# The last matmul of a feed-forward chain, with its operands' roles exchanged: 9 matmuls of 512 columns become 12 of 384

## What is computed

```python
def _moe2_ref(x, w1, w2, w3, w_out):      # x 3072 x 384, w1 and w2 384 x 1024
    a = x @ w1
    b = x @ w2
    h = a * b @ w3                        # w3 1024 x 1024
    return (h @ w_out).astype(np.float32) # w_out 1024 x 384
```

## Time and profile before

| | |
|---|---|
| median of 3 runs | 1001.33 us (1001.08 to 1002.03) |
| the profiled execution | 1001.33 us |
| its span, first to last instruction | 999.6 us |
| TensorE matmuls, busy | 903.1 us, 90% of the span, 5298 matmuls |
| VectorE, ScalarE, GpSimd busy | 608.0, 427.8, 70.0 us |
| the last block, from its first matmul to the end of the span | 700.9 to 999.6 us |

### The profile page before, as it was taken

One profiled execution on the slowest core, in us unless ns is written; L12 is line 12 of the kernel. 1 busy time (PEld: TensorE's weight loads), 2 busy tenths in 40 slices (PEclk: granted clock), 3 DMA queues, 4 the chain that ended last, 5 costly groups with the idle time before them and its releaser, 6 DMA issues.

```text
span 999.6 us, 14220 instructions
## 1 busy us (share of the span) xinstructions
PE 903.1 (90%) x5298; PEld 807.0 (81%) x5298; DVE 608.0 (61%) x974; ACT 427.8 (43%) x612; POOL 70.0 (7%) x56
## 2 busy tenths in 40 slices
PE   0964839999999899999899999988999999999998
PEld 0533739889989899899899999988788888888887
DVE  5977878989898898899899733345221212121211
ACT  3152264574674664764764654667011111112111
POOL 0000000000000000000000000000222222222221
PEclk9995669999999999999999999999999999999999
DMA  9666066273381470570660540142101010101000
GB/s 337 233 199 180 20 193 128 96 173 89 117 199 45 140 204 13 155 192 14 176 170 12 152 103 11 33 167 78 34 1 64 1 63 0 63 0 64 1 32 32
DMA packets 97878, 99.50 MB, mean 100 GB/s; under 512 B 6928, under 2 KB 88848, under 8 KB 97808
## 3 DMA queue, kind: packets, MB, share of 16 engines
q1 hardware_dynamic: 97808, 98.59, 34.5%
HBM read 63.96 MB, written 29.88 MB: 94 GB/s over the span
## 4 chain that ended last, share of the span: by engine, by line
PE 62%; DVE 22%; DVEq 6%; ACT 4%; issue 3%; DMA 2%; ACTq 1%; SPq 0%
PE ps_p L1285 8%; PE ps_p L1286 7%; PE ps_p L1287 7%; PE ps L1285 7%; PE ps L1287 7%; PE ps L1286 7%; PE ps_ay L1321 3%; DVE sp L1166 3%; DVE an L998 2%; PE ps_ay L1285 2%; PE ps_ay L1287 2%; PE ps_ay L1286 2%; PE ps_k L1285 2%; PE ps_k L1287 2%; PE ps_k L1286 2%
## 5 line engine op out<-in xcount | busy, mean ns | idle before, releaser
L1285 PE MATMUL ps_p<-x1h,win_h 128*128 128x384 f32 x336 | 118.3, 352 | 20.1 <-DVE sp L1166 20.1
L629 POOL TENSOR_TENSOR abl<-ab,abh 128x512 fp32r<-128x512 f32 x48 | 69.0, 1438 | 922.7 <-DVE abh L1267 922.7
L1285 PE MATMUL ps<-g_h,wo_h 128*128 128x384 f32 x384 | 132.3, 345 | 0.0
L1287 PE MATMUL ps<-g_h,wo_l 128*128 128x384 f32 x384 | 129.0, 336 | 0.0
L1286 PE MATMUL ps<-g_l,wo_h 128*128 128x384 f32 x384 | 128.8, 335 | 0.0
L1286 PE MATMUL ps_p<-x1l,win_h 128*128 128x384 f32 x336 | 114.0, 339 | 0.0
L1287 PE MATMUL ps_p<-x1h,win_l 128*128 128x384 f32 x336 | 113.9, 339 | 0.0
L1321 PE MATMUL ps_ay<-stq,stk 96*128 96x128 f32 x384 | 56.7, 295 | 37.5 <-DVE am L1120 15.2
L745 ACT ACTIVATE g_h<-sp 128x768 fp32r<-128x768 f32 (+1 forms) x71 | 55.4, 781 | 74.1 <-DVE sp L1166 74.1
L1258 DVE TENSOR_TENSOR ab<-ps_ay,bc 128x512 f32<-128x512 f32 x24 | 16.6, 692 | 114.6 <-ACT bc L894 114.6
L1321 PEld LDWEIGHTS ps_ay<-stq,stk 96*128 96x128 f32 x384 | 54.0, 208 | 38.8 <-issue 23.1
(11 more groups left out here) (140 smaller groups left out, 1997.2 us busy)
## 6 DMA issues: line engine op xcount, KB each, us to landing
qk_scr<-tt SPq DMA_DIRECT2D x16, 576.0 KB, 4.6
stq<-qk_scr SPq DMA_DIRECT2D x48, 192.0 KB, 4.9
qk_scr<-pp SPq DMA_DIRECT2D x16, 576.0 KB, 4.2
stk<-qk_scr SPq DMA_DIRECT2D x48, 192.0 KB, 4.6
an<-in_a_re SPq DMA_DIRECT2D x8, 576.0 KB, 4.1
an<-in_a_im SPq DMA_DIRECT2D x8, 576.0 KB, 5.1
qk<-in_q SPq DMA_DIRECT2D x8, 576.0 KB, 7.9
qk<-in_k SPq DMA_DIRECT2D x8, 576.0 KB, 8.8
```

Of the source, the lines that this page charges most:

```text
L629: tensor_tensor(abl[:, m % AR, :], ab[:, m % 2, :], abh[:, m % AR, :].bitcast(F32), ALU.subtract).then_inc(ab_lo, 1)
L1285: mm(o, wh, xh, start=start, stop=False)
L1287: return mm(o, wl, xh, start=False, stop=stop)
```

## The change

In the last matmul of the last block the operands exchange their roles: `abh` or `abl`, cut to 128 tokens, is the stationary operand, and the whole row block of W34 (384 columns) moves. For each step m there are 4 token blocks `s_` of 3 matmuls instead of 3 channel groups of 3. The output now comes out as tokens by channels, in four banks of which 384 columns are used; the fourth is `ps_ay[:, 1]`, which the last block did not use. ScalarE evicts 4 pieces of 384 columns per tile instead of 3 of 512, the semaphores `o_mm` and `o_ev` count in fours, the stores write rows of 384 channels (1536 bytes) instead of rows of 512 tokens (2048 bytes), and the host's reordering is another.

```diff
-        ost, _ = sb("ost", [P, 2, G, T2], at=at_g)
+        ost, _ = sb("ost", [P, 2, 4, DM], at=at_g)
...
-        ps_o = [ps_2[:, mo, :] for mo in range(G)]
+        ps_o = [ps_2[:, 0, 0:DM], ps_2[:, 1, 0:DM], ps_2[:, 2, 0:DM],
+                ps_ay[:, 1, 0:DM]]
...
             def store(t, u):
-                wait(o_ev, G * t + G + G)
-                eng.dma_start(out_c[:, :, bass.ts(t, T2)], ost[:, u, :, :]).then_inc(o_wr[u], 16)
+                wait(o_ev, 4 * t + 4 + 4)
+                eng.dma_start(out[bass.ts(t, T2), :].rearrange("(s p) n -> p s n", p=P),
+                              ost[:, u, :, :]).then_inc(o_wr[u], 16)
...
-            for mo in range(G):
-                wait(o_ev, G * (NT2 - 1) + mo + 1 + G)
-                eng.dma_start(out_c[:, mo, bass.ts(NT2 - 1, T2)], ost[:, 1, mo, :]).then_inc(o_wr[1], 16)
+            for s_ in range(4):
+                wait(o_ev, 4 * (NT2 - 1) + s_ + 1 + 4)
+                eng.dma_start(out[T2 * (NT2 - 1) + P * s_:T2 * (NT2 - 1) + P * s_ + P, :], ost[:, 1, s_, :]).then_inc(o_wr[1], 16)
...
-                for mo in range(G):
-                    eng.wait_ge(o_mm, G * t + mo + 1 + G)
-                    if mo == 0:
+                for s_ in range(4):
+                    eng.wait_ge(o_mm, 4 * t + s_ + 1 + 4)
+                    if s_ == 0:
                         eng.wait_ge(o_wr[u], 8 * t + (16 if u == 0 else 8))
-                    act(ost[:, u, mo, :], ps_o[mo], ACT.Copy).then_inc(o_ev, 1)
+                    act(ost[:, u, s_, :], ps_o[s_], ACT.Copy).then_inc(o_ev, 1)
...
-                        eng.wait_ge(o_mm, G * t + G)
+                        eng.wait_ge(o_mm, 4 * t + 4)
...
-                for mo in range(G):
+                for s_ in range(4):
                     if m == 0:
-                        eng.wait_ge(o_ev, G * t + mo + 1)
-                    ms = slice(P * mo, P * mo + P)
-                    last = mm3(ps_o[mo], w34h[:, m, ms], w34l[:, m, ms], abh[:, m % AR, :], abl[:, m % AR, :],
-                               m == 0, m == NM2 - 1)
+                        eng.wait_ge(o_ev, 4 * t + s_ + 1)
+                    ts = slice(P * s_, P * (s_ + 1))
+                    ah, al = abh[:, m % AR, ts], abl[:, m % AR, ts]
+                    mm(ps_o[s_], ah, w34h[:, m, :], start=m == 0, stop=False)
+                    mm(ps_o[s_], ah, w34l[:, m, :], start=False, stop=False)
+                    last = mm(ps_o[s_], al, w34h[:, m, :], start=False, stop=m == NM2 - 1)
```

More of the change, by code:

```diff
@@ L594, in _ @@
                 load_x2(0, 0)
-            out_c = out.rearrange("(g p) t -> p g t", p=P)
             def store(t, u):
-                wait(o_ev, G * t + G + G)
-                eng.dma_start(out_c[:, :, bass.ts(t, T2)], ost[:, u, :, :]).then_inc(o_wr[u], 16)
+                wait(o_ev, 4 * t + 4 + 4)
+                eng.dma_start(out[bass.ts(t, T2), :].rearrange("(s p) n -> p s n", p=P),
+                              ost[:, u, :, :]).then_inc(o_wr[u], 16)
             load_x2(1, 1)
@@ L607, in _ @@
             store(NT2 - 2, 0)
-            for mo in range(G):
-                wait(o_ev, G * (NT2 - 1) + mo + 1 + G)
-                eng.dma_start(out_c[:, mo, bass.ts(NT2 - 1, T2)], ost[:, 1, mo, :]).then_inc(o_wr[1], 16)
+            for s_ in range(4):
+                wait(o_ev, 4 * (NT2 - 1) + s_ + 1 + 4)
+                eng.dma_start(out[T2 * (NT2 - 1) + P * s_:T2 * (NT2 - 1) + P * s_ + P, :], ost[:, 1, s_, :]).then_inc(o_wr[1], 16)
             wait(o_wr[0], 16 * NT2 // 2 + 16)
-            wait(o_wr[1], 16 * NT2 // 2 + 16 + (G - 1) * 16)
+            wait(o_wr[1], 16 * NT2 // 2 + 16 + 3 * 16)
         @block.gpsimd
@@ L641, in _ @@
             eng.sem_inc(x2_ev, G)
-            eng.sem_inc(o_ev, G)
+            eng.sem_inc(o_ev, 4)
             def raw_high(i):
@@ L1289, in _ @@
             eng.sem_inc(ab_free, NM2 - 1)
-            eng.sem_inc(o_mm, G)
+            eng.sem_inc(o_mm, 4)
             eng.sem_inc(g_free, 1)
@@ L1519, in tokens_in_order @@
     def tokens_in_order(x):
-        x = np.asarray(x).reshape(DM, B * S // CT, RUN, CT // RUN)
-        return np.ascontiguousarray(x.transpose(1, 3, 2, 0).reshape(B * S, DM))
+        x = np.asarray(x).reshape(B * S // CT, RUN, CT // RUN, DM)
+        return np.ascontiguousarray(x.transpose(0, 2, 1, 3).reshape(B * S, DM))
     arrays = {name: channels_by_tokens(inputs[name]) for name in ("a_re", "a_im", "q", "k")}
@@ L1539 @@
     aps["w34_scr"] = nc.dram_tensor("w34_scr", (NM2, P, DM), F32, kind="Internal").ap()
-    aps["out"] = nc.dram_tensor("out_0", (DM, B * S), F32, kind="ExternalOutput").ap()
+    aps["out"] = nc.dram_tensor("out_0", (B * S, DM), F32, kind="ExternalOutput").ap()
     build(nc, **aps)
```

## The result

The changed kernel takes 1007.41 us (median of 6 runs, 1006.17 to 1008.5) against 1001.68 us for the kernel before (6 runs, 1000.57 to 1004.73). The ratio is 1.0052, with a 95% interval of 1.0036 to 1.0068: 3.6 to 6.8 us slower. The forecast was 1003.1 us and no change that can be measured. It was wrong: the time lies above its range of 1002.0 to 1004.1 us, and the whole interval of the ratio lies above 1.

The account below looks back on a forecast made before the run. TensorE's stream, never idle in the last block, was taken as the bound. Matmuls +1.92, last eviction -0.11 and last store -0.05 gave +1.76 us on 1001.33, so 1003.1 us, range 1002.0 to 1004.1.

Parts of the forecast that it names:

- What bounds the kernel: Last block: TensorE is never idle, so whatever the change adds to its stream is paid in full.
- Part 1, the matmuls: `down2`: 12 matmuls of 173.3 ns replace 9 of 226.7, 40 ns per step, +1.92 us over 48 steps.
- Part 2, the weight loads: `down2`: 12 loads instead of 9 per step, of about 188 ns, overlap the matmuls; cost 0.
- The rival for it: `down2`: weight loads become the bound, 188 ns per matmul, +10.4 us in all, 1011.5 us; chance 0.06.
- the 2.2 named as the sign of this rival: A `down2` above 2.2 us would show that weight loads bound it; the forecast had 2.08 us.
- Parts 3 to 5: Last block: operands ready in time, four evictions per tile hidden, changed semaphore counts and stores; cost 0 each.
- Part 6, the end: After the last matmul: last eviction -0.11 us, last store -0.05 us; the matmul's shorter duration already in the sum.
- Rival 1: `down2`: cost goes with columns alone, 170.0 ns per 384 columns, only the end changes, 1001.2 us; chance 0.07.
- Rival 3: Tile's turn: TensorE waits for the fourth eviction, paying what exceeds the cover of 3.1 us; chance 0.02.
- Rival 4: Unchanged earlier stages shift with the longer program, up to about 1 us either way; chance 0.10.
- The other constant: TensorE stream: the skill page's 2.5 ns rest per matmul; the added 144 matmuls would cost 0.36 us.

Follow-up runs that it names:

- e5: The changed kernel with 512 instead of 384 moving columns in its exchanged `down2`; 6.80 us per step, every distance 226 or 227 ns.
- e7: The kernel before with tiles of 384 tokens, old roles, every matmul of the last block with 384 columns; 1007.11 us, ratio 1.0050.
- e8: The changed kernel with tiles of 384 tokens, exchanged roles, every matmul of the last block with 384 columns; 1006.73 us, ratio 1.0057.
- e2: The changed kernel with two `up2` and then two `down2` in a row, half as many changes of column count; 1005.71 us, ratio 1.0030.
- e3: The changed kernel with each step cut in two, twice as many changes of column count; 1011.39 us, ratio 1.0088.
- e4: The kernel before, old roles, with `down2`, eviction and store cut to 384 of 512 tokens; 5.71 us per step.
- e6: The kernel before with `down2` cut to 448 of 512 tokens; 5.93 us per step.
- e9: The kernel before with `down2` cut to 256 of 512 tokens; 5.18 us per step.

## Why the prediction was wrong

- *What bounds the kernel*: right. TensorE has no idle time in the block in either kernel, so each nanosecond of its stream counts.
- *Part 1, the matmuls: here it failed.* The sum 12 x 173.3 - 9 x 226.7 took each distance from a stretch where all matmuls had the same size, and added them as if a stretch of one size followed another for nothing. The constant of 13.3 ns per matmul was right (e5, e7 and e8 have it to the nanosecond), and so was its 1.92 us. A changeover between sizes was no term of the sum at all: it stood at nothing, without a reason. What is missing is the price of 91 changes of size, 3.03 us, shown by the steps after and by e2, e3 and e4. By the stamps `down2` takes 2.106 us and not 2.080, but the larger part lies where I didn't look because the change doesn't edit it: `up2` takes 4.121 us instead of 4.080.
- A sign of it could have been found in the kernel before. The softplus block has matmuls of the attention between its own, and I had taken my row from a stretch without them. The timeline of before where matmuls of 384 columns follow those of the attention (96 x 128 and 96 x 96):

```profile
608.99 0.49 PE L1324 MATMUL ps_k<-ident,stk 96*128 96x96 f32 x4
609.27 0.42 PE L1285 MATMUL ps<-g_h,wo_h 128*128 128x384 f32 x1
609.52 0.34 PE L1286 MATMUL ps<-g_l,wo_h 128*128 128x384 f32 x1
...
610.23 0.33 PE L1287 MATMUL ps<-g_h,wo_l 128*128 128x384 f32 x1
...
610.92 0.33 PE L1285 MATMUL ps<-g_h,wo_h 128*128 128x384 f32 x1
```

  From 609.52 the first four distances sum to 0.71 us, the next four to 0.69; and the duration is 0.34 there and 0.33 later, the same mark as in the block after. By the stamps the first two are 176 and 182 ns and the rest regular: 12 ns too much, a warning and not the size of the price. The last block itself has 232, 233 and 231 ns after the clock's rise, ahead of the stretch from which the prediction took its 226.7 ns.
- *Part 2, the weight loads*: no price, right. The rival for it named one of the two places: it needed only 173.8 ns per matmul instead of 173.3 to pass 0.2%, and `down2` had 175.5 on average. It missed `up2`, gave the wrong mechanism (e6, e7) and, as its full size, 10.4 us. The measured `down2` of 2.11 us also lies between the forecast's 2.08 and the 2.2 named as the sign of this rival, so none of the signs covers what happened.
- *Parts 3 to 5* (operands ready, evictions hidden, counts and stores): right. After, the fourth eviction ends at 761.84, 3.4 us before TensorE comes back to the first of the banks (765.28) and 5.0 before it comes to the fourth:

```profile
759.85 1.47 ACT L885 ACTIVATE ost<-ps 128x384 f32<-128x384 f32 x3
761.35 0.49 ACT L885 ACTIVATE ost<-ps_ay 128x384 f32<-128x384 f32 x1
```

- *Part 6, the end*: right in sign, somewhat small. From the last matmul's start to the end of the span it is 0.30 us shorter; the prediction's terms for that stretch were 0.06 + 0.11 + 0.05 = 0.22. The last store lands in 1.9 instead of 2.1 us.
- *Rival 1* (cost by columns alone) is excluded by e7: 173.3, not 170.0 ns. *Rival 3* didn't occur. *Rival 4*, a shift of the earlier stages, I had bounded by 1 us; the block's start anywhere between 700.8 and 703.4 us in eleven profiles says that it can be more. It makes 0.54 us in the profiled execution and can't be told from chance in the medians.
- *The other constant*: the Trainium skill, page "TensorE: Matmul & The Clock Gate", section "Back-to-back issue gap", has N/2.4 + 2.5 ns for the gap of an isolated matmul. It would have made part 1 smaller still. The regular stretches of all runs here have 13.3 ns in place of the 2.5.

Put together, 1.97 + 3.03 - 0.30 is +4.7 us, inside both intervals, 3.6 to 6.8 and 2.8 to 5.2 us.

**What stays open.** Why the price of a change is 0, 73, 53, 67, 20 and 20 ns for the counts above is not known, and neither is what makes the distances irregular. The same series after the clock's rise (e5, e8) and after a wait (e3) suggests a stream that takes some matmuls to settle, but that is argued and not shown. The recorded weight loads give no hint: in regular and irregular stretches of the changed kernel alike each starts 2 to 4 ns after the matmul ahead of its own, and lasts 187 or 188 ns. Every matmul here has its own load, so no run tells what a stream without them would do. No version that does the whole computation beat the kernel before. Fewer changes of size in the softplus block would be the next thing to try there; its attention matmuls would have to lie together, and their waits on each other's results may stand against that. It was not tried.

## What to carry to other kernels

A matmul's price from a uniform stretch holds for a uniform stretch. Where a change mixes two sizes in a full TensorE stream, count the places where the size changes as instructions of their own (here 0 to 73 ns a pair), look in the trace right behind such places rather than in the middle of a run, and sum up the part that is not edited as well. At equal columns fewer and longer matmuls win (13.3 ns each here), and if sizes must be mixed, group them: two and two steps together gave half of the price back (12.387 us for two steps instead of 12.453).

## What was not expected of the hardware

- A change of the moving columns between 512 and 480, 448, 384, 320 or 256 makes up to nine of the next distances irregular, by 20 to 73 ns a pair of changes; with 496 columns there is no such price. In the changed kernel every steady step repeats it within 1 ns.
- The same series of irregular distances (231 to 236 ns among them at 512 columns, 175 to 185 at 384) also follows the clock's rise in e5 and e8 and a wait in e3, with one size of matmul.
- Steps in which the stationary blocks of `down2` have 96 instead of 128 columns take 40 ns more, at the same 512 moving columns.
- At the upper clock each of these matmuls, with a weight load of its own, costs 0.4167 ns per column and 13.3 ns, for 256 up to 512 columns (120 and 226.7 ns in the regular part of e9).
